# Attention ahead of a mixture of experts: TensorE's program as one loop with blank units ahead, and x copied aside by GpSimd and stored behind all the loads

## What is computed

```python
for c in range(nc):                       # 24 chunks of 32 queries in each of 4 batches
    q_c = q[:, :, c_start:c_end]
    k_full = np.concatenate([mem_k, k[:, :, l_start:r_end]], axis=2)   # 8 + 16 + 32 + 8 keys
    v_full = np.concatenate([mem_v, v[:, :, l_start:r_end]], axis=2)
    scores = scale * np.matmul(q_c, k_full.transpose(0, 1, 3, 2))
    a = np.exp(scores - np.max(scores, axis=-1, keepdims=True))
    a = a / (np.sum(a, axis=-1, keepdims=True) + 1e-09)
    out[:, :, c_start:c_end] = np.matmul(a, v_full)
...
logits = x @ w_gate                       # then: greedy assignment, experts, second block
```

## Time and profile before

| | us |
|---|---|
| median of 3 runs | 798.73 (794.93 to 800.34) |
| the profiled execution | 797.4 |
| its span in the profile | 795.6 |

### The profile page before, as it was taken

The page is one execution under the profiler, slowest core; times in us unless marked ns, Lnnn a source line. Parts: engine busy times, 40 slices in busy tenths (PEclk is TensorE's granted clock), DMA queues, the critical chain, the costliest instruction groups (busy, mean ns, idle before and its releaser), DMA issues.

```text
span 795.6 us, 17918 instructions
## 1 busy us (share of the span) xinstructions
PE 704.5 (89%) x7016; PEld 612.3 (77%) x7017; DVE 558.5 (70%) x2061; ACT 356.6 (45%) x567; POOL 303.0 (38%) x221
## 2 busy tenths in 40 slices
PE   3779986359979999899999998999999999999993
PEld 2557664248969888888979897988898989898882
DVE  3458776688688878777887788688869787741150
ACT  2558666424147325622571356136514741563270
POOL 2000001867057207721761375147514740672001
PEclk9999998569999999999999999999999999999997
DMA  8989986142133013301330232033103311330001
GB/s 232 286 252 291 302 251 226 57 145 78 33 104 108 36 53 107 106 28 54 111 102 28 82 106 78 28 93 120 54 29 118 119 54 52 106 108 28 0 14 40
DMA packets 24386, 83.89 MB, mean 105 GB/s; under 512 B 4033, under 2 KB 4097, under 8 KB 24321
## 3 DMA queue, kind: packets, MB, share of 16 engines
q0 software_dynamic: 13056, 46.14, 18.0%
q1 hardware_dynamic: 11264, 36.91, 15.2%
HBM read 70.46 MB, written 12.58 MB: 104 GB/s over the span
## 4 chain that ended last, share of the span: by engine, by line
PE 64%; DVE 11%; POOL 7%; issue 6%; DMA 6%; ACT 3%; SPq 1%; POOLq 0%; DVEq 0%; ACTq 0%
PE bank L574 18%; PE bank L576 16%; PE bank L575 16%; POOL wl L1388 4%; DMA raw<-w,w_idx 4%; PE bank L496 2%; PE banks L478 2%; DMA vr<-v_in 2%; DVE z L1206 2%; PE bank L453 2%; PE bank L463 2%; POOL raw L1382 1%; PE bank L489 1%; PE banks L603 1%; DVE hits L1027 1%
## 5 line engine op out<-in xcount | busy, mean ns | idle before, releaser
L1388 POOL TENSOR_TENSOR wl<-raw,wh 128x1024 fp32r<-128x1024 f32 x60 | 145.1, 2420 | 20.3 <-ACT wh L789 18.9
L1382 POOL DMA_INDIRECT raw<-w,w_idx x60 | 66.2, 1103 | 158.4 <-DVE w_idx L1121 121.4
L574 PE MATMUL bank<-xh,wh 128*128 128x384 f32 x256 | 90.4, 353 | 3.5 <-POOL wl L1388 3.3
L574 PE MATMUL bank<-hh,wh 128*128 128x384 f32 x256 | 90.0, 351 | 0.0
L576 PE MATMUL bank<-xh,wl 128*128 128x384 f32 x256 | 86.7, 339 | 0.0
L575 PE MATMUL bank<-xl,wh 128*128 128x384 f32 x256 | 86.5, 338 | 0.0
L576 PE MATMUL bank<-hh,wl 128*128 128x384 f32 x256 | 85.8, 335 | 0.0
L575 PE MATMUL bank<-hl,wh 128*128 128x384 f32 x256 | 85.8, 335 | 0.0
L789 ACT ACTIVATE wh<-raw 128x1024 fp32r<-128x1024 f32 x60 | 63.3, 1056 | 46.2 <-DMA raw<-w,w_idx 46.0
L574 PE MATMUL bank<-wout_h,uh 128*128 128x512 f32 x192 | 78.7, 410 | 0.2
L574 PE MATMUL bank<-win_h,yh 128*128 128x512 f32 x192 | 77.2, 402 | 0.0
(11 more groups left out here) (207 smaller groups left out, 1649.4 us busy)
## 6 DMA issues: line engine op xcount, KB each, us to landing
unit<-qk_in SPq DMA_DIRECT2D x24, 768.0 KB, 9.6
vr<-v_in SPq DMA_DIRECT2D x48, 130.0 KB
x_rows<-x_sb SPq DMA_DIRECT2D x24, 256.0 KB, 6.8
prep_first<-w_in SPq DMA_DIRECT2D x4, 512.0 KB, 5.9
vr<-v_mem SPq DMA_DIRECT2D x32, 32.5 KB
prep_first<-w_out SPq DMA_DIRECT2D x2, 512.0 KB, 8.1
prep_rest<-w_out SPq DMA_DIRECT2D x2, 512.0 KB, 9.0
raw<-w,w_idx POOLq DMA_INDIRECT x60, 4.3
```

The lines of the kernel that those rows point to most:

```text
L574: nc.tensor.matmul(bank, stat_h, mov_h, start=first, stop=False)
L1382: gp.indirect_dma_start(stage(s, c), None, table, bass.IndirectOffsetOnAxis(ap=w_idx[:, c % WCH:c % WCH + 1], axis=0))\
L1388: gp.tensor_tensor(wl[:, c % WCH, :], stage(s, c), wh[:, c % WCH, :].bitcast(F32), ALU.subtract)\
```

## The change

Three things are changed, all in the attention stage.

1. PE's program has no written-out steps at the start: the loop runs six passes instead of five, from step 0 on. The parts that don't exist yet in the steps 0 to 2 (probs_T(-1), values(-1), x_T(-2), x_T(-1), gate(-3) to gate(-1)) are done on zeros. DVE writes these zeros ahead of its own program, and all counts of semaphores are moved by a few (`BLANK_...`).
2. GpSimd copies each of the first 20 tiles of x from the ring `x_sb` to a buffer of its own, `x_keep`, and normalise(u) waits for that copy, where it waited for the store.
3. SP's loop over u holds loads only. All 24 stores stand behind it, 20 from `x_keep` and four from `x_sb`, and ahead of the eight loads of w_in and w_out.

```diff
@@ sync @@
             def load_v(u):
-                if u >= DEEP:
-                    sp.wait_ge(pv_ps, u - DEEP + 1)
+                if u >= DEEP - 1:
+                    sp.wait_ge(pv_ps, u - DEEP + 2)
...
             def store(u):
-                sp.wait_ge(x_ready, u + 1)
-                sp.dma_start(x_dram[u * P:u * P + P, :], x_sb[:, u % DEEP, :, :, :].rearrange("p a b d -> p (a b d)"))\
-                  .then_inc(x_stored[u % DEEP], 16)
+                if u < KEPT:
+                    sp.wait_ge(x_kept, u + 1)
+                    rows = x_keep[:, u, :]
+                else:
+                    sp.wait_ge(x_ready, u + 1 + BLANK_X)
+                    rows = x_sb[:, u % DEEP, :, :, :].rearrange("p a b d -> p (a b d)")
+                sp.dma_start(x_dram[u * P:u * P + P, :], rows).then_inc(x_stored[u % DEEP], 16)
...
                     load_v(u + DEEP)
+            for u in range(NT):
                 store(u)
-            sp.wait_ge(pv_ps, NT)
+            sp.wait_ge(pv_ps, NT + 1)
@@ tensor @@
-            def scores(u, r, n):
+            def scores(i, r, n):
                 pe.wait_ge(qk_loaded[r], 16 * n)
-                if not (isinstance(u, int) and u < 2):
-                    pe.wait_ge(shifted, u - 1)
-                if not (isinstance(u, int) and u < 4):
-                    pe.wait_ge(gate_sb, u - 3)
+                pe.wait_ge(shifted, i - 1 + BLANK_SHIFTED)
+                pe.wait_ge(gate_sb, i - 3 + BLANK_GATE)
...
                 if not known or i < NT:
                     scores(i, r, n)
-                if not known or 1 <= i <= NT:
-                    probs_T(i - 1, (r - 1) % DEEP)
-                if not known or i >= 3:
-                    gate(i - 3, (r - 3) % DEEP)
-                if not known or 2 <= i <= NT + 1:
-                    x_T(i - 2, (r - 2) % DEEP)
-                if not known or 1 <= i <= NT:
-                    values(i - 1, (r - 1) % DEEP)
+                if not known or i <= NT:
+                    probs_T(i, (r - 1) % DEEP)
+                gate(i, (r - 3) % DEEP)
+                if not known or i <= NT + 1:
+                    x_T(i, (r - 2) % DEEP)
+                if not known or i <= NT:
+                    values(i, (r - 1) % DEEP)
...
-            for i in range(DEEP):
-                step(i, i, 1)
-            with pe.Fori(1, NT // DEEP) as b:
+            with pe.Fori(0, NT // DEEP) as b:
                 for r in range(DEEP):
                     step(b * DEEP + r, r, b + 1)
@@ vector @@
+            ve.sem_inc(shifted, BLANK_SHIFTED)
+            nc.vector.memset(pr[:, 1, :, :, :], 0.0).then_inc(probs, 1)
+            nc.vector.memset(xT[:, 1, :, :], 0.0).then_inc(xT_sb, 1)
+            nc.vector.memset(x_sb[:, 2, :, :, :], 0.0).then_inc(x_ready, 1)
+            nc.vector.memset(pT[:, :, :, :], 0.0).then_inc(pT_sb, BLANK_PT)
+            nc.vector.memset(vr[0:64, RING - CPT:RING, :, :], 0.0).then_inc(v_next[0], 1)
+            nc.vector.memset(vr[64:128, RING - CPT:RING, :, :], 0.0).then_inc(v_next[1], 1)
+            nc.vector.memset(xT[:, 0, :, :], 0.0).then_inc(xT_sb, BLANK_XT - 1)
+            nc.vector.memset(x_sb[:, 3, :, :, :], 0.0).then_inc(x_ready, 1)
...
-                if n is not None:
-                    ve.wait_ge(x_stored[u % DEEP], 16 * n)
-                    ve.wait_ge(xT_ps, u - DEEP + 1)
+                if u >= DEEP:
+                    ve.wait_ge(x_kept, u - DEEP + 1)
+                if u >= 2:
+                    ve.wait_ge(xT_ps, u - 1)
@@ gpsimd @@
+            for u in range(KEPT):
+                gp.wait_ge(x_ready, u + 1 + BLANK_X)
+                gp.tensor_copy(x_keep[:, u, :], x_sb[:, u % DEEP, :, :, :].rearrange("p a b d -> p (a b d)")).then_inc(x_kept, 1)
```

More of the change, by code:

```diff
@@ L51 @@
 RING = DEEP * CPT
+KEPT = NT - DEEP
+BLANK_PT, BLANK_X, BLANK_XT, BLANK_SHIFTED, BLANK_GATE = 2, 2, 3, 2, 4
 TG = 12
@@ L167, in build @@
         below = sb("below", [P, 1], I32)
+        kept = ExitStack()
+        x_keep = sb("x_keep", [P, KEPT, DM], F32, kept)
+        kept.close()
         raw = sb("raw", [P, 2, 1024], F32)
@@ L199, in build @@
         x_ready = sem("x_ready")
+        x_kept = sem("x_kept")
         xT_ps = sem("xT_ps")
@@ L374, in next_front @@
             engine.wait_ge(v_loaded[(u + 1) % DEEP], v_count(u + 1))
-            if u >= DEEP:
-                engine.wait_ge(pv_ps, u - DEEP + 1)
+            if u >= DEEP - 1:
+                engine.wait_ge(pv_ps, u - DEEP + 2)
             own, after = slice(64 * a, 64 * a + FRONT), slice(64 * a + CHUNK, 64 * a + CHUNK + FRONT)
@@ L456, in scores, with probs_T @@
                 mm.then_inc(scores_ps, 1)
[L458 to L461, removed]
+            def probs_T(i, r):
+                pe.wait_ge(probs, i + 1)
+                pe.wait_ge(pT_sb, i - 1 + BLANK_PT)
                 for hp in range(HP):
@@ L465, in probs_T, with values @@
                 mm.then_inc(pT_ps, 1)
-            def values(u, r):
-                pe.wait_ge(pT_sb, u + 1)
+            def values(i, r):
+                pe.wait_ge(pT_sb, i + BLANK_PT)
                 for a in range(2):
-                    pe.wait_ge(v_next[a], u + 1)
-                if not (isinstance(u, int) and u < 1):
-                    pe.wait_ge(x_ready, u)
+                    pe.wait_ge(v_next[a], i + 1)
+                pe.wait_ge(x_ready, i - 1 + BLANK_X)
                 pe.sem_inc(pe_past, 1)
@@ L482, in values, with x_T @@
                 mm.then_inc(pv_ps, 1)
[L484 to L487, removed]
+            def x_T(i, r):
+                pe.wait_ge(x_ready, i - 1 + BLANK_X)
+                pe.wait_ge(xT_sb, i - 2 + BLANK_XT)
                 for k in range(KD):
@@ L491, in x_T, with gate @@
                 mm.then_inc(xT_ps, 1)
-            def gate(u, r):
-                pe.wait_ge(xT_sb, u + 1)
+            def gate(i, r):
+                pe.wait_ge(xT_sb, i - 2 + BLANK_XT)
                 for k in range(KD):
@@ L521, in _ @@
                 step(i, i % DEEP, 0)
-            pe.wait_ge(gate_sb, NT)
+            pe.wait_ge(gate_sb, NT + BLANK_GATE)
             for t in range(NT):
@@ L755, in _ @@
         def _(act):
+            act.sem_inc(gate_sb, BLANK_GATE)
             for i in range(NT + 3):
                 if 1 <= i <= NT:
-                    act.wait_ge(pT_ps, i)
-                    if i >= 3:
-                        act.wait_ge(pv_ps, i - 2)
+                    act.wait_ge(pT_ps, i + 1)
+                    if i >= 2:
+                        act.wait_ge(pv_ps, i - 1)
                     nc.scalar.activation(pT[:, (i - 1) % 2, :, :].rearrange("p a q -> p (a q)"), PT_PS[:, :], ACT.Copy)\
@@ L953, in soften @@
                 ve.wait_ge(row_max, u + 1)
-                if not (isinstance(u, int) and u < 2):
-                    ve.wait_ge(pT_ps, u - 1)
+                if u >= 1:
+                    ve.wait_ge(pT_ps, u)
                 for a in range(2):
@@ L960, in soften, with normalise @@
                 last.then_inc(shifted, 1)
-            def normalise(u, r, n):
+            def normalise(u, r):
                 pv = PW[:, :, 0:HP * (D + 1)].rearrange("p a (h d) -> p a h d", h=HP)
-                ve.wait_ge(pv_ps, u + 1)
+                ve.wait_ge(pv_ps, u + 2)
                 nc.vector.tensor_scalar(rs[:, r % 2, :, :], pv[:, :, :, D], 1e-9, None, ALU.add).then_inc(row_sum, 1)
@@ L979, in _ @@
                 if u >= 1:
-                    normalise(u - 1, (u - 1) % TPB, None if u - 1 < DEEP else (u - 1) // DEEP)
+                    normalise(u - 1, (u - 1) % TPB)
                 next_front(ve, lambda to, of: nc.vector.tensor_copy(to, of), 0, u)
-            normalise(NT - 1, TPB - 1, NT // DEEP - 1)
+            normalise(NT - 1, TPB - 1)
             ve.wait_ge(consts, 2)
```

11 lines of the change are left out of this document (5 added, 6 removed).

## The result

| | median, us | lowest and highest | runs |
|---|---|---|---|
| before | 799.22 | 794.93 to 803.7 | 14 |
| after | 793.17 | 788.7 to 799.97 | 14 |

The ratio is 0.9929, with a 95% interval of 0.9906 to 0.9952: the change saves 5.7 us (3.8 to 7.5), about half of the 10.5 that I had summed up. The profiled execution of after took 793.11 us, its span is 791.4.

A forecast was written before the change was run, and what follows sets the result against it. It took PE's program fetches to bound attention's start and the queue of loads and stores its middle; -6.5 - 5 + 0 + 1 = -10.5 us from 797.4 gave 786.9, stated as 787.5 us, range 778 to 795.

The forecast's parts named there:

- One loop: Start of attention: half the blocks to fetch saves 6.7 us of stall, less 1.7 for blank units: net 5 us saved.
- cover: Start of attention: PE's idle for the second tile and first value unit, 4.2 us, hides part of the blank units.
- blanks: Steps 0 to 2: PE's units done on zeros take 5.5 us at the granted clock of most of this stage.
- rival A: Start of attention: fewer fetched blocks, each late, cost as much stall as before; 792 us, chance 0.13.
- Stores behind the loads: Steps 8 to 23: queue falls from 4.5 to about 3.65 us a tile, below PE's need; 6.5 us saved.
- DVE's zeros: Kernel start: DVE writes the zeros while idle before the first scores; 0 to 3 us, taken as 0.
- GpSimd's copies: Attention steps: 20 copies of at most 1.16 us each fit within a step of 3.71; cost 0.
- rival B: Attention steps: DVE's ring copy waits for GpSimd's copy, up to 1.16 us in 20 steps; 806 us, chance 0.07.
- The tail: Search after attention: late w_in puts GpSimd's low parts beside other DVE work, stalling it; +1 us net.
- C: Start of attention: all stalls but one block's go and the clock stays up; 779 us, chance 0.10.
- D: Search: stores end late and w_in lands later than 7 us, 2 to 4 us on top; 790 us, chance 0.07.
- E: PE's loop: each jump back fetches its target anew, about 5 us at the longest stall; 792 us, chance 0.03.

The follow-up runs named there:

- loop_only: The changed kernel with the stores put back among the loads and without GpSimd's copies: 794.01 us, ratio 0.995 to before.
- behind_only: The kernel before with only GpSimd's copies and the stores behind all loads, PE's first steps still written out: 796.82 us, ratio 0.9983.
- stores_twice: The kernel before with every store made a second time, to another DRAM buffer, 6.3 MB more: 802.78 us, ratio 1.0072.
- w_in_first: The changed kernel with 12 of the 24 stores ahead of the loads of w_in and w_out and 12 behind: 787.54 us, ratio 0.9872 to before.
- no_copies: The changed kernel without GpSimd's 20 copies, the stores taking zeros: 791.0 us, ratio 0.9885 to before.
- no_memory: The changed kernel without the 24 small loads of memory values for tiles 6 to 21, 0.8 MB: 789.72 us, ratio 0.9879 to before.
- memory_64_rows: The changed kernel with those 24 memory loads written as 64 rows of 520 bytes to 64 partitions of a scratch buffer: 788.39 us, ratio 0.9865.

## Why the prediction was right or wrong

- **What bounds the stretches.** Right for the start, which waited for its program. Wrong for the middle in one point: the stores were taken as a part of the queue's work in proportion to their bytes.
- **One loop, -5.0.** Measured -5.2 in after, -4.9 in loop_only, and a ratio of 0.995 for it alone. Its working was less good than its sum: I had stalls -6.7, cover -4.2 and blanks +5.5, with 0.4 for the clock. The rows show stalls -3.4 (13.4 to 10.0), cover -4.2, and in net only 2.5 us more of busy PE. Half the fetches took three quarters of the stall, so each became dearer (2.5 us a block, before 1.7), which is half of what rival A had, and the small rise of busy PE made it up. The blanks themselves weren't cheap. By their starts in after they took 8.0 us, where I had 5.5, and the granted clock of the stretch fell from 0.97 to 0.88. So the real units of the stretch took less than before, for which no term stood: the second tile's scores took 0.85 us, before 1.17. That the term came out right is luck.
- **Stores behind the loads, -6.5.** This step failed. Measured: -2.0 in after's profile; -3.4 as the mean of four executions of the same steps (65.5, 63.0, 63.0, 65.1); -5.7 in behind_only's one profile, where the start was 1.4 us longer. The term rested on "301 GB/s was measured with the same mix of loads in it", and so priced loads alone at 3.65 us a tile, just under PE's 3.71. But a rate of a mix isn't the rate of its parts. The stores cost 4.4 us for 6.3 MB (stores_twice), not 21. The loads move at 262 to 281 GB/s without them in these four executions, which is 4.2 to 3.9 us a tile, over PE's 3.71. The lower bound that I had set beside it, "nothing, if the loads alone already need over 4.2 us a tile", was nearly the case in after, and it had been given no rival of its own.
- **DVE's zeros, 0.** PE's first scores came at 6.39 us (before 6.50), and no row shows a wait for them. Right.
- **GpSimd's copies, 0, and rival B.** They take 1.13 us in the median, in a step of 3.7, and DVE's ring copy kept its 0.69 us in the median. B's cost falls, and no_copies left the middle where it was. The race that B describes does take place. Mostly DVE's copy starts first and GpSimd's lasts 1.14 us instead of 0.62; DVE's longest copy went from 0.69 us to 0.95. From after, one such pair, then all copies by duration (min/median/max ns):

```profile
59.25 0.69 DVE L999 COPY vr<-vr 24x1040 f32<-24x1040 f32 x1
59.28 1.14 POOL L1385 COPY x_keep<-x_sb 128x512 f32<-128x512 f32 x1 [2.56 <-DVE x_sb L991]
...
L1385 POOL COPY x_keep<-x_sb x20: 616/1132/1138, 20.2 to 105.5; 128x512 f32<-128x512 f32 x20
...
L999 DVE COPY vr<-vr x30: 275/692/947, 12.5 to 117.0; 24x1040 f32<-24x1040 f32 x18, 24x780 f32<-24x780 f32 x6, 24x260 f32<-24x260 f32 x6
```

- **The tail, +1.** Right in kind, too small in size: two instructions were held for 2.2 us each, inside the bounds of -1.6 to +5, and the search grew by 2.6. w_in_first took it back. GpSimd started 3.1 us later than before, where I had at most 6: the stores were priced at 301 GB/s here too, and from 116 to 123 us, with stores in the queue, it moved 376. The Trainium skill ("GPSIMD Engine Reference", Key points) names DVE instructions with two SBUF inputs among those that contend with GpSimd. The trace agrees for L1146, which reads two tensors and was held. L1139, held as well, reads one tensor and a scalar for each partition; L1142 between them reads one tensor and took 0.14 us.
- **Rivals C, D, E.** C needs the start shorter by 11.7: no. D: GpSimd started 8.2 us behind the logits, not over 12, and still waited 7.5 us for the row numbers: no. E: no packet on q8 between 51 and 116 us, with three jumps back in it, and loop_only is faster than before: no. So the rule of the Trainium skill ("Runtime: NRT & Kernel Launch", Instruction fetch mechanics) that I weighed there has no cost for this loop.
- **The sum.** -5.2 - 2.0 + 2.6, and +0.4 of the rest, give -4.2 for the two spans. With the mean of the four middles it is -5.6, and the medians show -6.0 (-5.7 by the ratio). The forecast of 787.5 us is what w_in_first reached, but by a smaller term for the stores and none for the tail: a coincidence.

## What to carry to other kernels

A queue's rate measured on a mix of loads and stores can't be shared out by bytes: before costing a store (or a load) at its bytes, look for a stretch without it, or double it once and measure. Look also at the smallest transfers in a full queue, and at how many partitions each fills, before the large ones. And when transfers are moved behind others, put what another engine waits for ahead of what nobody waits for: w_in ahead of half or all of the stores gave 2 to 2.5 us in the search and 4 to 6 by the ratios, beside the 5.7 of the change itself.

## What the hardware showed that I had not expected

- Stores of 2 KB rows among loads were nearly free: 6.3 MB more cost 4.4 us, 0.7 us a MB (0.9 by the ratio), where loads cost 3.8 (262 GB/s).
- 0.8 MB of loads in rows on eight partitions cost 4 to 5 us by the ratios (after 0.9929, no_memory 0.9879, memory_64_rows 0.9865). The same bytes as 64 rows on 64 partitions cost no time that shows, with the queue just as full (100.4%).
- The same program's full queue moved 244 GB/s in one execution and 278 in another, and this stretch made nearly the whole difference of 8 us between them.
- A VectorE instruction of 0.23 us took 2.26 because GpSimd's instruction was running, and the one of 0.36 us took 2.21.
- TensorE's loop body, 576 matmuls and as many weight loads in four steps, was fetched once for six passes.
